# Attention, a dense layer and eight routed experts on one core: the hand-over from expert 0 to expert 1 is reordered

## The reference

```
logits = x @ w_gate                      # x: 1536 x 384, 8 experts
expert_idx = np.argmax(logits, axis=1)   # each token goes to one expert
...                                      # disp[e] = its tokens, in order, up to capacity 384
h = np.maximum(np.einsum('ecd,edf->ecf', disp, w1), 0.0)   # 384 -> 1024, relu
y = np.einsum('ecf,efd->ecd', h, w2)                        # 1024 -> 384
out[i] = gate_w[i] * y[expert_idx[i], pos[i]]
```

## Time and profile before

| | |
|---|---|
| median of 3 runs | 416.16 us (414.52 to 416.44) |
| profiled execution, its own time | 414.46 us |
| its span, first to last instruction | 412.7 us |
| PE busy | 401.9 us |
| DVE, POOL, ACT busy | 250.5, 234.1, 188.3 us |
| granted TensorE clock, mean | 0.997 |

### The profile page before, as it was taken

How to read it: one execution, slowest core, us unless ns; L and a number is a source line. 1 busy time by engine, 2 the same in 40 slices (tenths; PEclk the granted TensorE clock), 3 DMA queues, 4 the chain that set the end, 5 groups by cost and what they waited for, 6 DMA issues and landing times.

```text
span 412.7 us, 9450 instructions
## 1 busy us (share of the span) xinstructions
PE 401.9 (97%) x3655; PEld 386.0 (94%) x3655; DVE 250.5 (61%) x583; ACT 188.3 (46%) x409; POOL 234.1 (57%) x239
## 2 busy tenths in 40 slices
PE   8999999999999999999999999999889999999995
PEld 7799799999999999999999999998889999999995
DVE  7787955376566546654663487775567466475532
ACT  4786553233433333333343455443446465465520
POOL 3789865567865785578334335166072744746531
PEclk9999999999999999999999999999999999999998
DMA  7999996213130303020009001833767758668100
GB/s 279 404 395 348 349 373 248 75 46 111 49 119 2 139 21 119 2 87 21 2 2 361 3 2 38 302 102 67 307 191 220 248 175 307 183 201 270 69 33 28
DMA packets 26442, 64.99 MB, mean 157 GB/s; under 512 B 11787, under 2 KB 19509, under 8 KB 24224
## 3 DMA queue, kind: packets, MB, share of 16 engines
q1 hardware_dynamic: 24464, 59.68, 42.0%
q0 software_dynamic: 1792, 4.73, 3.0%
q10 hardware_dynamic: 144, 0.00, 0.0%
HBM read 51.98 MB, written 13.21 MB: 158 GB/s over the span
## 4 chain that ended last, share of the span: by engine, by line
PE 84%; DVE 6%; issue 4%; DMA 2%; ACT 2%; POOL 1%; SPq 0%; POOLq 0%; DVEq 0%; ACTq 0%
PE bank L1423 24%; PE bank L1425 24%; PE bank L1424 24%; PE bank L1444 2%; DMA we_raw<-wexp 2%; PE bank L1473 1%; PE bank L1509 1%; PE bank L1513 1%; PE bank L1502 1%; PE bank L1505 1%; DVE we_lo L1363 1%; PE bank L1600 1%; PE bank L1774 1%; PE bank L1686 1%; PE bank L1775 1%
## 5 line engine op out<-in xcount | busy, mean ns | idle before, releaser
L730 POOL TENSOR_TENSOR g_lo<-elu,g_hi 128x256 fp32r<-128x256 f32 x95 | 73.8, 778 | 87.2 <-ACT g_hi L913 86.6
L1423 PE MATMUL bank<-xt,wd_hi 128*128 128x256 f32 x285 | 80.5, 283 | 0.6 <-DVE elu L1228 0.6
L1425 PE MATMUL bank<-xt,wd_lo 128*128 128x256 f32 x285 | 80.4, 282 | 0.0
L1424 PE MATMUL bank<-xt,wd_hi 128*128 128x256 f32 x285 | 80.3, 282 | 0.0
L904 ACT ACTIVATE elu<-elu 128x256 f32<-128x256 f32 x96 | 40.1, 418 | 75.6 <-DVE elu L1220 75.1
L1423 PE MATMUL bank<-wd_hi,g_hi 128*128 128x392 f32 (+1 forms) x192 | 67.4, 351 | 0.0
L1425 PE MATMUL bank<-wd_hi,g_lo 128*128 128x392 f32 (+1 forms) x192 | 65.2, 340 | 0.0
L1228 DVE SCALAR_TENSOR_TENSOR elu<-elu,bank 128x256 f32<-128x256 f32 x96 | 40.2, 419 | 41.1 <-ACT elu L904 41.1
L1424 PE MATMUL bank<-wd_lo,g_hi 128*128 128x392 f32 (+1 forms) x192 | 65.1, 339 | 0.0
L913 ACT CAST g_hi<-elu 128x256 fp32r<-128x256 f32 x96 | 39.0, 406 | 44.0 <-DVE elu L1228 44.0
L1423 PEld LDWEIGHTS bank<-xt,wd_hi 128*128 128x128 f32 x285 | 53.9, 189 | 1.3 <-DVE elu L1228 1.1
(11 more groups left out here) (221 smaller groups left out, 947.8 us busy)
## 6 DMA issues: line engine op xcount, KB each, us to landing
we_raw<-wexp SPq DMA_DIRECT2D x8, 1536.0 KB, 9.0
wd_raw<-wexp SPq DMA_DIRECT2D x8, 1536.0 KB, 6.5
rkt<-rkt SPq DMA_DIRECT2D x12, 512.0 KB, 5.7
nat<-nat SPq DMA_DIRECT2D x9, 672.0 KB, 5.2
wd_raw<-win SPq DMA_DIRECT2D x4, 768.0 KB, 8.6
wd_raw<-wout SPq DMA_DIRECT2D x4, 768.0 KB, 8.9
wo_tr<-wouttr SPq DMA_DIRECT2D x1, 3072.0 KB, 17.5
slots<-blank SPq DMA_DIRECT2D x1, 2702.0 KB, 14.1
```

What stands on the lines that cost most here:

```text
L730: nc.gpsimd.tensor_tensor(g_lo[:, f % 4, :], elu[:, f % 2, :], g_hi[:, f % 4, :].bitcast(F32), ALU.subtract).then_inc(s_glo, 1)
L1423: mm(dst, w_hi, x_hi, start=start, stop=False)
L1424: mm(dst, w_hi, x_lo, start=False, stop=False)
L1425: return mm(dst, w_lo, x_hi, start=False, stop=stop)
```

## The change

Four edits, all between expert 0's second tile and expert 1's first groups. No matmul is added or left out, and no DMA.

1. VectorE: `tokens_of(1, s_tok[0])` moves from behind the late tile's last split to right behind `tokens_of(0, s_atok)`.
2. The late tile's second layer goes by quarters of 256 hidden features in place of halves of 512: each quarter has a PSUM bank of its own (4, 2, 5, 3), its own cast on ScalarE and subtraction on VectorE. Quarters 0 and 1, which need only half 0 of `hrow`, are turned one k-tile sooner; quarters 2 and 3 are turned behind the first two `tile_fc2`.
3. `tile_fc2(6)` and `tile_fc2(7)` move behind the first-layer groups 0 and 1 of expert 1; with them go the rise of `s_fc2e` and VectorE's `gated(1)`.
4. On ScalarE the cast of the last third of expert 1's W2 (`expert1_hi(N1 + 2)`) moves from ahead of the late tile's casts to behind them; `expert_x` stands between the second and third quarter. Expert 1's second layer no longer waits for `s_ye[0]`, since it writes other banks than the late tile does.

```diff
-        ps_ht = [bank[2:4], bank[4:6]]
+        ps_ht = bank[2:4]
+        ps_hq = [bank[4], bank[2], bank[5], bank[3]]
...
+            def quarter_hi(q):
+                act.wait_ge(s_lht, q + 1)
+                nc.scalar.copy(ge_hi_tile[:, q * SN:(q + 1) * SN], ps_hq[q][:, 0:SN]).then_inc(s_gehi, ET // 4)
...
             tile_row(s_lh, s_lrow)
+            for q in range(2):
+                quarter_hi(q)
+            expert_x(0, 1)
+            for q in range(2, 4):
+                quarter_hi(q)
             expert1_hi(N1 + 2)
-            for b in range(2):
-                tile_hi(b, ps_ht[1], s_lht, s_gehi, ET // 2)
-            expert_x(0, 1)
...
+            def quarter_lo(q):
+                dve.wait_ge(s_gehi, ET // 4 * (q + 1))
+                cols = slice(q * SN, (q + 1) * SN)
+                V.tensor_tensor(ge_lo_tile[:, cols], ps_hq[q][:, 0:SN], ge_hi_tile[:, cols].bitcast(F32),
+                                ALU.subtract).then_inc(s_gelo, ET // 4)
...
             tokens_of(0, s_atok)
+            tokens_of(1, s_tok[0])
...
                     if f == 1 and not behind:
+                        dve.wait_ge(s_fc2e, ET)
+                        dve.wait_ge(s_tok[0], 1)
+                        gated(1, ps_y[0][:, 0:DM])
                         dve.wait_ge(s_ehi[1], 2 * N1)
...
             expert_cols(0, 1)
+            for q in range(2):
+                quarter_lo(q)
             tile_row(s_he, ET, s_lrow)
-            for b in range(2):
-                tile_lo(b, ps_ht[1], s_gehi, s_gelo, ET // 2)
+            for q in range(2, 4):
+                quarter_lo(q)
             expert_x(0, 1)
-            tokens_of(1, s_tok[0])
...
-            dve.wait_ge(s_fc2e, ET)
-            dve.wait_ge(s_tok[0], 1)
-            gated(1, ps_y[0][:, 0:DM])
             expert(0, 1, True, False)
...
+            def quarter_transpose(q):
+                pe.wait_ge(s_lrow[q // 2], 1)
+                for i in range(2):
+                    last = nc.tensor.transpose(ps_hq[q][:, i * C:(i + 1) * C],
+                                               hrow[:, q * SN + i * C:q * SN + (i + 1) * C], ident[:, :])
+                last.then_inc(s_lht, 1)
...
-                    if f == 0:
+                    if f == 0 and not (r == 1 and isinstance(i, int) and i == 0):
...
+                    if f < 2 and not behind:
+                        pe.wait_ge(s_gelo, ET)
+                        last = tile_fc2(ET - 2 + f)
+                        if f == 1:
+                            last.then_inc(s_fc2e, ET)
...
             tile_fc1(1, 1, 0, s_he, ET)
+            pe.wait_ge(s_pgt, 1)
+            for q in range(2):
+                quarter_transpose(q)
             tile_fc1(1, 1, 1, s_he, ET)
-            pe.wait_ge(s_pgt, 1)
-            tile_transpose(0, ps_ht[1], s_lrow, s_lht)
             tile_fc1(1, 1, 2, s_he, ET)
-            tile_transpose(1, ps_ht[1], s_lrow, s_lht)
             pe.wait_ge(s_ye[0], 1)
-            for f in range(ET):
-                if f % (ET // 2) == 0:
-                    pe.wait_ge(s_gelo, ET // 2 + f)
-                last = tile_fc2(f)
-            last.then_inc(s_fc2e, ET)
+            for f in range(ET - 2):
+                if f % 2 == 0:
+                    pe.wait_ge(s_gelo, f + 2)
+                tile_fc2(f)
+                if f == 1:
+                    for q in range(2, 4):
+                        quarter_transpose(q)
             expert(0, 1, True, False)
```

More of the change, by code:

```diff
@@ L950, in _ @@
             expert1_hi(0)
-            tile_hi(0, ps_ht[0], s_aht, s_aghi, 1)
+            tile_hi(0, ps_ht, s_aht, s_aghi, 1)
             expert1_hi(1)
@@ L955, in _ @@
                            ps_s[0][:, 0:DM].rearrange("p (k n) -> p k n", k=KT)).then_inc(s_xehi[0], 2)
-            tile_hi(1, ps_ht[0], s_aht, s_aghi, 1)
+            tile_hi(1, ps_ht, s_aht, s_aghi, 1)
             for c in range(2, N1 + 2):
@@ L1303, in _ @@
             tile_row(s_ah, 2, s_arow)
-            tile_lo(0, ps_ht[0], s_aghi, s_aglo, 1)
+            tile_lo(0, ps_ht, s_aghi, s_aglo, 1)
             dve.wait_ge(s_xehi[0], 2)
@@ L1310, in _ @@
             link(V.tensor_tensor(gt[0][:, 1, :], gt[0][:, 1, :], ps_s[1][:, 0:2], ALU.add))
-            tile_lo(1, ps_ht[0], s_aghi, s_aglo, 1)
+            tile_lo(1, ps_ht, s_aghi, s_aglo, 1)
             tokens_of(0, s_atok)
+            tokens_of(1, s_tok[0])
             for c in range(N1 - 1):
@@ L1707, in _ @@
             count(NB - 1)
-            tile_transpose(0, ps_ht[0], s_arow, s_aht)
+            tile_transpose(0, ps_ht, s_arow, s_aht)
             tile_fc1(0, 1, 2, s_ah, 1)
@@ L1729, in _ @@
             pick_rows()
-            tile_transpose(1, ps_ht[0], s_arow, s_aht)
+            tile_transpose(1, ps_ht, s_arow, s_aht)
             pe.wait_ge(s_elo1[0], 2 * N1)
```

## The result

The changed kernel takes 410.55 us (median of 6 runs, 410.47 to 410.59), where the kernel before, measured beside it, took 415.35 (6 runs, 414.52 to 416.44). The ratio is 0.9891, its 95% interval 0.9875 to 0.9908: faster by 1.1%. The forecast was 412.1 us, range 410.2 to 413.8. Against that median the gain is 3.9 us, against the six runs above 4.8.

The account below looks back on a forecast made before the run. PE bounds the kernel, idling in three waits around the late tile and expert 1. Removing them gives 1.0 from the late tile plus 3.0 from expert 1: 416.16 - 4.0 = 412.1 us, range 410.2 to 413.8.

Parts of the forecast that it names:

- Three waits, all in the hand-over: PE's only waits from 255 us on, 1.1, 1.0 and 0.8 us, lie between late tile's first layer and expert 2.
- Tokens, W1 in time: Early token cast lets SP issue W1 at 281.7, not 287.63; expert 1's ge_lo waits go, 3.0 us gained.
- the 14.68 of the sum: Expert 1's time without waits: two groups of first layer only at 1.04 and six full groups at 2.10.
- the hold: GpSimd's W2 split, started first at 300.76, holds VectorE's third W1 split: 3.08 us instead of 1.21.
- Late tile: Second layer by quarters: PE's 1.27 loss at hrow replaced by 0.16 + 0.10, a gain of 1.0 us.
- The wait of 1.27: PE before the late tile's second transposes, waiting for half 1 of hrow: 0.95 lost, plus 0.32 in slower transposes.
- The thin margins: Half 1 of hrow ready 0.1 before the second transposes, quarter 2 split before tile_fc2(4) at 284.06; a miss costs 0.1 to 0.5.
- That the terms add up: The late tile's 1.0 and expert 1's 3.0 were summed to 4.0 us less at expert 2's start, 300.84.
- Rule and race: VectorE and GpSimd splits take whole turns at the SBUF port; VectorE still starts first, near 274 and at its third W1 split.
- The second rival: Extra token cast makes VectorE lose the race at 274; PE waits 2.3, gain 1.7, 414.4 us; chance 0.06.
- W2: Expert 2's W2 issued at about 288.4, landing 295.1 to 299.5; lateness costs only from a landing at 299.0.
- the fast end: The profiled execution, 414.46, lies 1.7 below the 416.16 median; 1.7 below the 412.1 forecast was called the fast end.

Follow-up runs that it names:

- The first experiment: Kernel before with one edit, the second token cast moved right behind the first: 411.54 us, ratio 0.9928.
- the kernel with W1 held: Kernel before with the early token cast, plus the W1 load held until the late tile's second layer is done: 411.87 us, ratio 0.9956 against the kernel before.

## Why the prediction was right, point by point

- **Three waits, all in the hand-over.** Right: with them gone the span fell by 3.9 of the forecast 4.0, and expert 2's start came at 300.97 where 300.84 was worked out. By parts the trace gives 3.02 for expert 1 (17.72 to 15.76 and the 1.06 moved into it; forecast 3.04) and 0.90 for the late tile (8.23 to 6.27, less the 1.06; forecast 1.0).
- **Tokens, W1 in time.** Right: issue at 281.88 for 281.7. The first experiment gives the term alone 2.84. The prediction put all 3.04 of expert 1 to it; 0.13 to 0.18 of that is the cover by the moved groups (22.16 without them against 22.03, and 14.86 against the 14.68 of the sum). What it says of the cause, that the load was issued late, is half of it: in the kernel before this load took 7.51 us to its first use, more than the 6.9 at most of the earlier trace rows, and the kernel with W1 held shows that a late issue with a landing in 6.60 costs only 0.48 in expert 1 (15.34 for 14.86) where the hold does not come on top.
- **Late tile.** The wait of 1.27 is replaced by 0.25 of wait and transposes of 0.38, 0.27 in all, where 0.16 + 0.10 was put. The sum left out what the moved second transposes cost behind them, the 0.12 above; that is the 0.1 between the forecast 4.0 and the 3.9 measured. The thin margins held: `tile_fc2(4)` started at 284.11, with quarter 2 ready.
- **That the terms add up.** This step is the weakest. The sum reads as if the late tile's 1.0 could be had alone. Without the tokens it is worth nothing (ratio 0.9997), because W1's issue is then fixed by the cast at 285.2 on VectorE and PE only waits longer. The total was right since both edits were made.
- **Rule and race.** The two engines do take turns whole: at 274 (6.42 us for VectorE's two splits when GpSimd is first, 4.56 otherwise) and at 301 (3.08 or 1.21). This is what the Trainium skill states in "SBUF — State Buffer", section "SBUF: two separate sides"; the runs agree at both places, and with 2.40 in place of the prediction's 8.19/3 for GpSimd's first split the end at 301 comes out to 0.01 instead of 0.3. The second rival's price was 2.3 by its working and is 1.70. Counted from h, VectorE's two splits ended 2.45 later than in the changed kernel, where 2.7 was put. Of this 0.44 was made up before quarter 0 (its split began 2.01 later) and 0.35 more before PE stood still (1.66), since PE asks first for quarter 0 alone: 0.79 taken up, where 0.4 was put.
- **W2.** Right: issued at 288.70 for 288.4, landed in 6.5 us, and the price begins at a landing of 299.0.
- **The size in absolute terms.** 412.1 against 410.55. The difference of 4.0 was right and the base was off: 416.16 is the median of three runs, of which two, 416.16 and 416.44, lie above every one of the 68 runs taken later on three chips (median 414.47); whether that is chance or the chip is not shown. The prediction took its profiled execution, 414.46, for "the fast end"; it lies in the middle of the 68, and 414.46 - 4.0 = 410.5 is what was measured. That the time fell inside the range is owed to the 1.9 of spread that the range reached down. The 4.8 against the six runs beside the result, of which these three are half, is more than the 3.9 that the traces find for the edits.

## What to carry to other kernels

A load's issue time can hang on a small instruction that has nothing to do with it but stands ahead of it in the issuing queue; follow the queue's own waits, not only the data's, and ask how long the load then takes, since the cost hangs on the landing. A gain ahead of a fixed event is worth nothing until the event moves: fix what starts the late transfer first, then shorten the work before it. And where one kernel's runs spread by microseconds and another's do not, look for a late transfer on the path and for two engines that start near a tie behind it; don't take the median of three such runs for a base, and forecast from the trace's own parts. Here the gain was that of the trace, 3.9, against the middle of 68 runs.

## What the runs showed of the hardware that was not expected

- Six one-column memsets on VectorE, independent of each other, take up next to no time in its queue: the 1024-column split behind them started 0.18 us behind the two casts (273.75 to 273.93), as against 0.13 without them (273.95 to 274.08).
- The same 1.5 MB load took from issue to ScalarE's first read of it 7.51, 6.96, 8.08 and 6.92 us in the four traces in which row loads were issued right before it, and 6.60 in the one in which it was late without them. With one trace each, that the row loads do it is a guess.
